# An attention and feed-forward kernel: row products moved from VectorE to GpSimd, and a new order for the first pair

## What is computed

```python
def _attn_ref(q, k, v, M_prev, z_prev, beta):
    scores = scale * np.matmul(q, k.transpose(0, 1, 3, 2))
    scores = np.where(causal, -1000000000.0, scores)
    a = np.exp(scores - scores.max(-1, keepdims=True))
    a /= a.sum(-1, keepdims=True) + 1e-09
    local = np.matmul(a, v)
    q_p = phi(q)                    # where(x > 0, x, exp(x) - 1) + 1
    mem_ret = np.einsum('bhsd,bhde->bhse', q_p, M_prev)
    mem_norm = np.einsum('bhsd,bhd->bhs', q_p, z_prev)[..., None] + 1e-06
    g = 1.0 / (1.0 + np.exp(-beta))[None, :, None, None]
    return g * mem_ret / mem_norm + (1 - g) * local

x = attn_out as (tokens, 512)
x = f1(x @ w_in) @ w_out            # f1: 0 below -1, x above 1, (x + 1) ** 2 / 4 between
x = f2(x @ w_in2) @ w_out2          # f2: x * sigmoid(x)
```

## Time and profile before

| | |
|---|---|
| median of 3 runs | 987.01 us (986.19 to 989.4) |
| the profiled execution | 988.2 us, its span 986.1 us |
| mean granted TensorE clock | 0.997 of full |
| busy: TensorE, its weight loads | 975.1 us (99%), 816.0 us (83%) |
| busy: VectorE, ScalarE, GpSimd | 474.3, 384.1, 285.6 us |
| moved by DMA | 48.10 MB |

### The profile page before, as it was taken

How to read it: one execution, slowest core, us unless ns; L and a number is a source line. 1 busy time by engine, 2 the same in 40 slices (tenths; PEclk the granted TensorE clock), 3 DMA queues, 4 the chain that set the end, 5 groups by cost and what they waited for, 6 DMA issues and landing times.

```text
span 986.1 us, 14130 instructions
## 1 busy us (share of the span) xinstructions
PE 975.1 (99%) x5468; PEld 816.0 (83%) x5468; DVE 474.3 (48%) x946; ACT 384.1 (39%) x847; POOL 285.6 (29%) x304
## 2 busy tenths in 40 slices
PE   7999999999999999999999999999999999999998
PEld 6888877888888888888888998888888888888897
DVE  6999999756344434434434663323332332322232
ACT  6988888633223222322223332322222232222232
POOL 6989999799000000000000798000000000000000
PEclk8999999999999999999999999999999999999999
DMA  6555544244000000000000343001000100100010
GB/s 196 150 157 154 168 145 131 71 119 117 22 1 1 1 0 1 1 1 1 1 1 1 86 129 97 0 1 43 1 1 1 44 0 1 43 1 1 1 44 22
DMA packets 38401, 48.10 MB, mean 49 GB/s; under 512 B 3264, under 2 KB 21696, under 8 KB 38336
## 3 DMA queue, kind: packets, MB, share of 16 engines
q1 hardware_dynamic: 38336, 47.20, 15.9%
HBM read 42.47 MB, written 4.72 MB: 48 GB/s over the span
## 4 chain that ended last, share of the span: by engine, by line
PE 83%; DVE 8%; POOL 3%; issue 2%; ACT 2%; DMA 1%; SPq 0%; POOLq 0%; DVEq 0%
PE ps L1021 26%; PE ps L1023 26%; PE ps L1022 26%; PE ps L899 2%; PE ps L954 1%; DVE prob L653 1%; DVE qlo L635 1%; PE ps L862 1%; DVE ptail L653 1%; DVE mden L659 1%; DVE rw L685 1%; POOL phir L358 1%; ACT prob L476 1%; DVE glo L797 1%; POOL phs L386 1%
## 5 line engine op out<-in xcount | busy, mean ns | idle before, releaser
L1021 PE MATMUL ps<-xhi,W 128*128 128x512 f32 (+1 forms) x640 | 235.4, 368 | 0.0
L1022 PE MATMUL ps<-xlo,W 128*128 128x512 f32 (+1 forms) x640 | 235.4, 368 | 0.0
L1023 PE MATMUL ps<-xhi,W 128*128 128x512 f32 (+1 forms) x640 | 235.4, 368 | 0.0
L797 DVE TENSOR_TENSOR glo<-act_t,ghi 128x512 fp32r<-128x512 f32 (+1 forms) x160 | 118.0, 738 | 223.6 <-ACT ghi L576 223.6
L576 ACT CAST ghi<-act_t 128x512 fp32r<-128x512 f32 (+1 forms) x160 | 92.5, 578 | 235.4 <-PE ps L1023 213.1
L1021 PEld LDWEIGHTS ps<-xhi,W 128*128 128x128 f32 x640 | 120.7, 189 | 20.7
L1022 PEld LDWEIGHTS ps<-xlo,W 128*128 128x128 f32 x640 | 120.6, 188 | 20.4
L1023 PEld LDWEIGHTS ps<-xhi,W 128*128 128x128 f32 x640 | 120.6, 188 | 20.2
L335 POOL CAST W<-stage 128x512 fp32r<-128x512 f32 x64 | 46.2, 722 | 303.0 <-PE ps L1023 300.6
L568 ACT ACTIVATE act_t<-act_t,half_col 128x512 f32<-128x512 f32 (+1 forms) x80 | 54.5, 681 | 185.7 <-DVE act_t L790 185.7
L1021 PE MATMUL ps<-ghi,W 128*128 128x512 f32 (+1 forms) x320 | 118.1, 369 | 0.3 <-DVE glo L797 0.2
(11 more groups left out here) (113 smaller groups left out, 1336.5 us busy)
## 6 DMA issues: line engine op xcount, KB each, us to landing
stage<-in_moe_w_in SPq DMA_DIRECT2D x32, 256.0 KB, 2.7
stage<-in_moe_w_out SPq DMA_DIRECT2D x32, 256.0 KB, 2.7
vn<-in_vN SPq DMA_DIRECT2D x16, 320.0 KB, 5.0
qraw<-in_qT SPq DMA_DIRECT2D x15, 320.0 KB, 3.2
qn<-in_qN SPq DMA_DIRECT2D x16, 288.0 KB, 4.9
zb<-in_zN SPq DMA_DIRECT2D x32, 144.0 KB, 3.6
out_x<-ostage SPq DMA_DIRECT2D x17, 256.0 KB, 2.0
kraw<-in_kT SPq DMA_DIRECT2D x15, 288.0 KB, 2.9
```

The lines of the kernel that those rows point to most:

```text
L797: nc.vector.tensor_tensor(glo[:, f % SLOTS, 0:TN[tile]], a, ghi[:, f % SLOTS, 0:TN[tile]].bitcast(F32), ALU.subtract).then_inc(glo_done, 1)
L1021: nc.tensor.matmul(dst, w_lo_, x_hi_, start=first, stop=False)
L1022: nc.tensor.matmul(dst, w_hi_, x_lo_, start=False, stop=False)
L1023: return nc.tensor.matmul(dst, w_hi_, x_hi_, start=False, stop=last)
```

## The change

Each pair's three small products of two SBUF operands leave VectorE for GpSimd: `shares` (gate times reciprocal, into a tile of its own, `share`) and `weights` (rw, rwt) stand ahead of `weigh`. VectorE keeps den, the two reciprocals and the sum. In pair 0 TensorE's scores run all high x high and low-k products of s = 0, 2, 3 first, with three warm-up products where six were; ScalarE rounds `khi` and `qhi` of pair 1, GpSimd makes `klo` and `qlo` of it and both its phi sums; ScalarE puts two exponentials ahead of pair 0's phi, and copies of pair 0 ahead of pair 1's exponentials.

```diff
@@ -39,7 +39,7 @@
     FIRST_AT = ((TILES - 2, 14), (TILES - 2, 14), (TILES - 2, 15), (TILES - 1, 4))
     SCALE = 1.0 / float(D) ** 0.5
     EARLY = 4
-    WARM = 6
+    WARM = 3
     NB = 2 * FULL + 1
     MAIN = FULL * P
     assert 2 * D == P and PAIRS == KC and TN[-1] == 2 * P and TAIL == D and FULL == 4
@@ -379,8 +381,23 @@
                 nc.gpsimd.tensor_copy(rwide[:, 0:2 * FULL, :], rw[:, 0, 0:2 * FULL].unsqueeze(2)
                                       .broadcast_to([P, 2 * FULL, D])).then_inc(row_wide, 1)
 
+            def shares(p):
+                pool.wait_ge(norm_step, 2 * p + 2)
+                if p == 0:
+                    pool.wait_ge(gate_step, 5)
+                nc.gpsimd.tensor_tensor(share[:], mden[:, 1], gcols[:, p % PAIRS, :], ALU.mult).then_inc(gated, 1)
+
+            def weights(p):
+                pool.wait_ge(gated, p + 1)
+                pool.wait_ge(row_step, 2 * p + 1)
+                nc.gpsimd.tensor_tensor(rw[:, 1, :], den[:], share[:], ALU.mult).then_inc(row_made, 1)
+                pool.wait_ge(row_step, 2 * p + 2)
+                pool.wait_ge(row_made, 2 * p + 1)
+                nc.gpsimd.tensor_tensor(rwt[:], rw[:, :, 2 * FULL:].broadcast_to([P, 2, 2]),
+                                        bd[:].unsqueeze(1).broadcast_to([P, 2, 2]), ALU.mult).then_inc(row_made, 1)
+
             def weigh(p):
-                pool.wait_ge(row_step, 4 * p + 4)
+                pool.wait_ge(row_made, 2 * p + 2)
                 if p:
                     pool.wait_ge(t_full, TURNS * (p - 1) + T_PHI + 1)
                 nc.gpsimd.tensor_tensor(phs[:, 0:2 * FULL, :], phir[p % 3][:, 0:2 * FULL, :],
@@ -416,10 +433,12 @@
                 nc.gpsimd.memset(bd[e * D:(e + 1) * D, e:e + 1], 1.0).then_inc(made, 1)
             pool.wait_ge(made, 13)
             nc.gpsimd.tensor_tensor(sident[:], ident[:, 0:D], ident[:, D:P], ALU.add).then_inc(made, 1)
-            high_k(1)
-            high_q(1)
-            pool.wait_ge(hi_done, 3)
+
+            pool.wait_ge(second_high, 1)
+            nc.gpsimd.tensor_tensor(klo[1][:], k_raw(1), khi[1][:].bitcast(F32), ALU.subtract).then_inc(second_low, 1)
+            pool.wait_ge(second_high, 2)
             nc.gpsimd.tensor_tensor(qlo[1][:], q_raw(1), qhi[1][:].bitcast(F32), ALU.subtract).then_inc(second_low, 1)
+            pool.sem_inc(hi_done, 2)
             phi_sum_1(0)
             phi_sum_2(0)
             phi_times_z(0)
@@ -427,17 +446,21 @@
             for p in range(NPAIR):
                 if 0 < p < NPAIR - 1:
                     phi_sum_1(p + 1)
+                shares(p)
+                weights(p)
                 weigh(p)
                 widen(p)
 
                 for u in parts_beside(p):
                     split_part(u)
-
                 if 0 < p < NPAIR - 1:
                     phi_sum_2(p + 1)
                 if p + 2 < NPAIR:
                     high_k(p + 2)
                     high_q(p + 2)
+                if p == 0:
+                    phi_sum_1(1)
+                    phi_sum_2(1)
                 if p + 1 < NPAIR:
                     phi_times_z(p + 1)
                     weigh_v(p + 1)
@@ -452,6 +475,10 @@
             nc.scalar.copy(qhi[0][:], qraw[:]).then_inc(first_q, 1)
             act.wait_ge(b_in, 32)
             nc.scalar.activation(gate[:, 0, :], braw[:], ACT.Exp, scale=-1.0).then_inc(gate_exp, 1)
+            act.wait_ge(k_in[1], 16)
+            nc.scalar.copy(khi[1][:], k_raw(1)).then_inc(second_high, 1)
+            act.wait_ge(q_in[1], 16)
+            nc.scalar.copy(qhi[1][:], q_raw(1)).then_inc(second_high, 1)
 
             def phi_part_1(p):
                 act.wait_ge(n_in[p % 2], 16 * (p // 2 + 1))
@@ -508,13 +535,14 @@
                 act.wait_ge(t_full, TURNS * p + T_ROW + 1)
                 nc.scalar.copy(turned[:, 1, 0:MAIN], ring(p, T_ROW)).then_inc(ev_act, 1)
 
+            for c in range(2):
+                exps(0, c)
             phi_part_1(0)
             phi_part_2(0)
-            for c in range(6):
+            for c in range(2, 6):
                 exps(0, c)
 
-            act.wait_ge(lo_done, 3)
-            act.wait_ge(second_low, 1)
+            act.wait_ge(second_low, 2)
             empty_first(0)
             for c in range(6, NB):
                 exps(0, c)
@@ -529,6 +557,8 @@
                 empty_main(p, T_M20, 2, 0)
                 if p == 0:
                     empty_main(0, T_M30, 3, 0)
+                    empty_main(0, T_M31, 3, 1)
+                    empty_tail(0)
                 if made_here < NPAIR:
                     phi_part_2(made_here)
                 if more:
@@ -536,15 +566,19 @@
                     exps(p + 1, 1)
                 if p:
                     empty_main(p, T_M30, 3, 0)
-                if more:
+                if p and more:
                     exps(p + 1, 2)
                     exps(p + 1, 3)
-                empty_main(p, T_M31, 3, 1)
-                empty_tail(p)
-                if more:
+                if p:
+                    empty_main(p, T_M31, 3, 1)
+                    empty_tail(p)
+                if p and more:
                     exps(p + 1, 4)
                 empty_rest(p)
                 empty_phi(p)
+                if p == 0:
+                    for c in range(2, 5):
+                        exps(1, c)
                 empty_row(p)
                 if not more:
                     for k_ in range(KC):
@@ -657,35 +691,23 @@
                 if step == 0:
                     dve.wait_ge(phi_norm, p + 1)
                     nc.vector.tensor_reduce(mden[:, 0], phie[p % 2][:], AX.X, ALU.add).then_inc(norm_step, 1)
-                elif step == 1:
-                    dve.wait_ge(norm_step, 3 * p + 1)
+                else:
+                    dve.wait_ge(norm_step, 2 * p + 1)
                     if p:
-                        dve.wait_ge(row_step, 4 * p - 1)
+                        dve.wait_ge(gated, p)
                     nc.vector.reciprocal(mden[:, 1], mden[:, 0]).then_inc(norm_step, 1)
-                else:
-                    dve.wait_ge(norm_step, 3 * p + 2)
-                    dve.wait_ge(gate_step, 5)
-                    nc.vector.tensor_tensor(mden[:, 1], mden[:, 1], gcols[:, p % PAIRS, :],
-                                            ALU.mult).then_inc(norm_step, 1)
 
             def rows(p, step):
                 if step == 0:
                     dve.wait_ge(exp_done, NB * p + NB)
+                    if p:
+                        dve.wait_ge(row_made, 2 * p)
                     nc.vector.tensor_scalar(den[:], rowsum[:, p % 2, :], 1e-9, None, ALU.add).then_inc(row_step, 1)
-                    return
-                dve.wait_ge(row_step, 4 * p + step)
-                if step == 1:
+                else:
+                    dve.wait_ge(row_step, 2 * p + 1)
                     if p:
                         dve.wait_ge(t_full, TURNS * p)
                     nc.vector.reciprocal(rw[:, 0, :], den[:]).then_inc(row_step, 1)
-                elif step == 2:
-                    dve.wait_ge(norm_step, 3 * p + 3)
-                    if p:
-                        dve.wait_ge(weighed, 2 * p)
-                    nc.vector.tensor_tensor(rw[:, 1, :], den[:], mden[:, 1], ALU.mult).then_inc(row_step, 1)
-                else:
-                    nc.vector.tensor_tensor(rwt[:], rw[:, :, 2 * FULL:].broadcast_to([P, 2, 2]),
-                                            bd[:].unsqueeze(1).broadcast_to([P, 2, 2]), ALU.mult).then_inc(row_step, 1)
 
             def split_x(layer, tile, k_):
                 tok = slice(T0[tile], T0[tile] + TN[tile])
@@ -723,19 +745,18 @@
                                   gate[:, 0, 0:2 * PAIRS].rearrange("p (k e) -> p k e", e=2).unsqueeze(2)
                                   .broadcast_to([P, PAIRS, FULL, 2])).then_inc(gate_step, 1)
             nc.vector.tensor_copy(gcols[:, :, 2 * FULL], gate[:, 0, 2 * PAIRS:]).then_inc(gate_step, 1)
-            low_k(1)
             dve.wait_ge(made, 6)
             for c in range(NB):
                 maximum(0, c)
 
-            dve.wait_ge(second_low, 1)
-            dve.sem_inc(lo_done, 1)
+            dve.wait_ge(second_low, 2)
+            dve.sem_inc(lo_done, 2)
             empty_second(0)
             dve.wait_ge(made, 14)
             for p in range(NPAIR):
                 more, more2 = p + 1 < NPAIR, p + 2 < NPAIR
                 if p:
-                    for step in range(4):
+                    for step in range(2):
                         rows(p, step)
                     if more:
                         to_x(p - 1)
@@ -762,10 +782,6 @@
                         maximum(p + 1, c)
                 if p == 0:
                     maximum(1, 8)
-                    dve.wait_ge(phi_part, 4)
-                    nc.vector.tensor_tensor(phir[1][:], qn[1][:], phir[1][:], ALU.add).then_inc(phi_sum, 1)
-                    dve.wait_ge(phi_sum, 3)
```

(32 more changed lines are left out.)

## The result

The changed kernel takes **990.64 us** (median of 14 runs, 989.86 to 991.02) where the kernel before takes 986.86 (14 runs, 985.96 to 989.40): a ratio of **1.0037, 95% interval 1.0030 to 1.0044**, or 3.8 us slower. The prediction was 988.6 us with "no change" as the likeliest; the time lies inside its range (984.0 to 991.5) but above its 990.0, so slower is what happened. The kernel before has two groups of runs, eight at 985.96 to 987.01 us and six at 987.96 to 989.40, and its median moves with their shares; the changed kernel has one. The profiled execution of after took 990.65 us, its span 988.6, against 988.2 and 986.1 before: 2.45 us more, and the execution traced before is of the upper group.

A forecast was written before the change was run, and what follows sets the result against it. Four engines near full bound attention, the slowest setting each pair; after the change GpSimd would. Removed stalls -3.7, new stalls +5.0 and start +0.3 gave +1.6 us on the 987.01 median: 988.6 us, range 984.0 to 991.5.

The forecast's parts named there:

- GpSimd becomes the bound: Steady attention pairs: GpSimd needs 23.26 us per two pairs against TensorE's 22.10, short by 1.16 us.
- 0.85 us a pair: GpSimd's cost for the three moved products, gaps included, in each attention pair; bounds 0.45 and 1.2 us.
- Pairs 7, 9, 11 and 13 lose 1.16 each: Weight-splitting pairs: late khi delays klo, 4.65 us; with 0.35 at pair 5, 5.0 us of stalls.
- -3.7 + 5.0: Steady pairs: 3.7 us of present stalls removed by unloading VectorE, 5.0 us of new stalls from GpSimd.
- GpSimd keeps up: Rival, chance 0.22: products near 0.45 us a pair, stalls only 1.0 to 1.5 us, time 983.5 to 984.8 us.
- GpSimd's queue decides for worse: Rival, chance 0.22: products cost 1.0 to 1.2 us a pair, stalls 6.7 to 8.6, time 990.3 to 992.2 us.
- The 0.35 us that I booked for the split of pair 5: Pair 5: GpSimd's phs is 1.9 us behind the mark, 0.35 over the 1.54 us allowed.
- all 16 den rows say otherwise: VectorE's den: mean 0.164 us, taken as evidence that tensor_scalar does not contend with GpSimd.
- the prediction's own signs of being wrong: Marks 11.05 apart throughout, stalls in pairs 2 to 4, den over 0.3 us, or pair 1's eleven before 30.0.
- So +0.3 us, between -0.9 and +0.8: Start, pairs 0 and 1: pair 1's eleven transposes come at about 30.9 instead of 30.6 us.
- the same 1.6: Sum: +1.6 us on the profiled 988.2 us, added equally to the median of 987.01, giving 988.6 us.
- The clock rival: Rival, chance 0.06: TensorE's clock stays at half behind 18.6 us too, up to 4 us more, 990 to 992.

The follow-up runs named there:

- the early start: Kernel before with 3 warm-up products in place of 6: 986.51 us, ratio 0.9999; its trace has a span of 984.6 us.
- the run without den: Changed kernel without the addition of 1e-9 to the row sums, which are used directly: 989.71 us, ratio 1.0034 to before.
- the trace with 6 warm-up products: Changed kernel with 6 warm-up products in place of its 3: 989.88 us, ratio 1.0034 to before.
- the trace with the first pair alone: Kernel before with the changed first pair and 3 warm-up products, row products left on VectorE: 989.74 us, ratio 1.0027.
- the one with the splits last: Changed kernel with all eight early weight splits on GpSimd beside pair 15, none beside pairs 5 to 14: 988.54 us, ratio 1.0016 to before.
- the two of the changed kernel with ScalarE's old order: Changed kernel with three pair 1 exponentials back ahead of pair 0's copies: 990.30 us; the same with all phi on VectorE from pair 1: 983.19 us.

## Why the prediction was right and wrong

**Right: the bound.** "GpSimd becomes the bound, short by 1.16 us in every two pairs": 1.23 by the trace (23.33 against 22.10 us). 0.85 us a pair for the three products was 0.91 to 0.93, the single product 0.20 to 0.25 was 0.20 to 0.22. "Pairs 7, 9, 11 and 13 lose 1.16 each" and 5.0 us in all: 1.13, 1.23, 1.23, 1.23 and 5.15. The last column grew by 1.46 us against the trace of before with the early start (164.91 - 163.45), by 1.86 against the profiled one (163.05), where -3.7 + 5.0 gave 1.3. The sum stopped at pair 14, which "feeds no further klo", and so left out the 0.4 us that are lost behind it. The rivals went out where they should: it is not "GpSimd keeps up", and the cost stayed under the 1.0 us from which "GpSimd's queue decides for worse" takes over. The 0.35 us that I booked for the split of pair 5 did not come; instead den made the 0.33 us of pair 4.

**Wrong reading: den.** "The scalar addition den at 128.63, inside the same GpSimd operation, takes 0.16" and "all 16 den rows say otherwise". It was not inside: den begins at 128.63 and phir at 128.65, 0.02 us later. In the kernel before, den stood behind the product mden x gcols, which itself had waited until GpSimd was between operations, so that none of the 16 den begins while a GpSimd operation still has more than 0.06 us to run. The change removed that product and exposed den: 1.33 us in pair 4, 0.71 in pair 0, 0.68 in pair 5 and about 0.3 in the rest. Two of the prediction's own signs of being wrong came with it, a den over 0.3 us and a stall in pairs 2 to 4. So the trace of after agrees with the rule set aside there, of the Trainium skill, SBUF — State Buffer, "Who interferes with whom", that tensor_scalar can enter a mode that contends. For the reciprocal, inside a GpSimd addition, the traces show 0.22 us and no wait. The error cost the sum almost nothing: with GpSimd the bound, what VectorE waits comes out of its idle time, as the run without den shows.

**Mis-sized term: the start.** "So +0.3 us, between -0.9 and +0.8." Against the profiled execution it was +0.69 (31.26 - 30.57), inside the bounds. Against the early start, which 8 of the 14 timed runs of before have by their times, it is **+2.56** (31.26 - 28.70; +1.7 in the trace with 6 warm-up products, where pair 0's own transposes came 0.86 earlier). The failed step is in the sum, where the median gets "the same 1.6" as the profiled execution. That execution had pair 0's second scores at half clock, so TensorE bound its start and hid what the new order costs; I took the 1.2 us between it and the median for a shift of the whole. Of the new first pair, ScalarE's order and GpSimd's phi sums bind pair 1 instead, 0.91 us each, and a longer time at half speed behind 12 us hardly moves them: the trace with the first pair alone, at half speed up to about 18 us, has its eleven transposes at 30.24, and the one with the splits last, at half speed up to about 15, at 30.34. Half speed in the first scores is another matter. The prediction put it at nothing, since the new wait for ScalarE would cover it; the trace of after had it and lies 0.85 us behind the one with 6 warm-ups, but the medians do not tell these two kernels apart. The sum by the traces is +2.56 + 1.46 = 4.0 us on the span (984.6 to 988.6); measured were 3.8 on the medians. Taken against the profiled execution it is +0.7 + 1.9 = 2.5 (986.1 to 988.6), and the rest is that this execution lay above its median. So the 1.6 us were right in direction, and the measured time is inside the range by the range's width. ScalarE's part was read rightly for the profiled execution: pair 0's third exponential starts at 11.16 us (before 11.11), and pair 1's last one ends at 27.24 ("about 27.2 as before"). TensorE, whose mark came at 26.06, waited 0.53 us for it; in the early start of before it ends at 25.11. The product phie x zb of pair 1 ended at 27.74 us (predicted 27.1), GpSimd's two additions taking 1.92 and 1.78 us, not 1.4:

```profile
22.45 1.92 POOL L355 TENSOR_TENSOR phir<-qn,phir 128x576 f32<-128x576 f32 x1
24.45 1.78 POOL L360 TENSOR_TENSOR phir<-phir,phie 128x576 f32<-128x576 f32 x1
26.31 1.43 POOL L365 TENSOR_TENSOR phie<-phir,zb 128x576 f32<-128x576 f32 x1
```

and VectorE idled for it:

```profile
27.77 0.76 DVE L693 TENSOR_REDUCE mden<-phie 128x9 f32<-128x585 f32 x1 [2.72 <-POOL phie L365]
```

**The clock rival** was out: the granted clock from 18.6 to 32 us was 1.00, and the warm-up products moved neither kernel's median clear of noise.

## What to carry to other kernels

Before moving work to an engine that seems to have room, add up its queue over the period in which its load repeats (here two pairs, one with a weight split): the engine at 148 of 160 us was the one to unload, and taking 3.1 us a pair of large sums off it for 0.76 us elsewhere gained 3.1 us, where moving 0.9 us of small ones onto it lost 1.95. An operation that shows no wait in any row may only stand behind one that waits for it; compare start times to the hundredth before saying what lies inside what. And when the profiled execution is not at the median, find out which stretch makes the difference before a term of that stretch is added to the median.

## What the runs showed of the hardware

- VectorE's tensor_scalar on 128x9 fp32, one SBUF operand, waits for a running GpSimd tensor_tensor: 1.33 us against 0.16. A reciprocal of the same shape does not (0.21 to 0.22 us inside one, 12 times in the changed kernel).
- GpSimd's two-operand product on 9 or 4 columns takes 0.20 to 0.22 us, and its next start comes 0.07 to 0.15 us after its end where one waits for the other.
- GpSimd's addition on 576 columns takes 1.41 us in some places and 1.92 in others, and VectorE's two-operand ones 0.75 or up to 1.24 (klo, 576 columns) and 2.04 (qlo, 640). The long ones overlap two-operand work of the other engine: phir of 1.92 us at 22.45 runs beside qlo of 2.04 at 23.02.
- TensorE's speed in the first 18 us differs between executions of the same code. In three traces (before with 3 warm-up products, and the two of the changed kernel with ScalarE's old order) the profile lists a granted clock of 1.00 from 5 to 18.6 us, while products run at half speed: two 64x512 ones take 0.63 us as late as 9.52 in the first and 16.33 in the second, and 0.40 at full speed; in the third six transposes take 1.79 us at 11.45, and 0.88 at full speed. The products' own durations are the surer sign of the clock there:

```profile
15.48 0.63 PE L872 MATMUL ps<-khi,qlo 64*128 64x512 f32 x2
15.90 0.63 PE L872 MATMUL ps<-klo,qhi 64*128 64x512 f32 x2
16.33 0.63 PE L872 MATMUL ps<-khi,qhi 64*128 64x512 f32 x2
```

These rows are of the changed kernel with ScalarE's old order, TensorE's timeline.
